# Masking attention scores in place in PSUM with a bitwise AND, in a linear attention kernel with two feed-forward layers

## What is computed

```python
for t in range(S):                       # attention, per batch and head
    kt, vt, rt, wt = (k[:, :, t], v[:, :, t], r[:, :, t], w[:, :, t])
    cur = np.einsum('bhd,bhe->bhde', u[None] * kt, vt)
    y[:, :, t] = np.einsum('bhd,bhde->bhe', rt, state + cur)
    state = wt[:, :, :, None] * state + np.einsum('bhd,bhe->bhde', kt, vt)
...
h = x @ w_in
g = np.maximum(h, 0.0) + alpha * np.minimum(h, 0.0)
x = g @ w_out
...
logits = x @ w_gate                      # then for each expert e, for its tokens:
h = np.maximum(xe @ w1[e], 0.0)
ye = h @ w2[e]
out[mask] = gate_w[mask, None] * ye
```

## Time and profile before

| | us |
|---|---|
| median of 3 runs | 925.89 (922.28 to 926.36) |
| profiled execution, its time | 920.69 |
| its span on the core | 919.0 |
| TensorE busy (matmuls) | 784.9 (85%) |
| VectorE busy | 559.2 (61%) |
| ScalarE busy | 440.3 (48%) |
| POOL busy | 410.0 (45%) |

### The profile page before, as it was taken

The page is one execution under the profiler, slowest core; times in us unless marked ns, Lnnn a source line. Parts: engine busy times, 40 slices in busy tenths (PEclk is TensorE's granted clock), DMA queues, the critical chain, the costliest instruction groups (busy, mean ns, idle before and its releaser), DMA issues.

```text
span 919.0 us, 19098 instructions
## 1 busy us (share of the span) xinstructions
PE 784.9 (85%) x6487; PEld 498.6 (54%) x6488; DVE 559.2 (61%) x1077; ACT 440.3 (48%) x826; POOL 410.0 (45%) x384
## 2 busy tenths in 40 slices
PE   3568979979988988997997997993999999999992
PEld 0364556557556556556556556551555565555551
DVE  8788787787788678868868868213333333333330
ACT  1655756755764763773773773741222222222320
POOL 5305856854963872883973874651001011110100
PEclk9789989999998998998998998996999999999997
DMA  8645552543434335326327324696543415424110
GB/s 256 218 134 133 165 162 75 170 142 96 136 128 144 111 130 168 101 92 213 101 70 229 103 75 148 238 321 230 217 144 95 164 35 183 170 52 166 49 35 14
DMA packets 43372, 128.96 MB, mean 140 GB/s; under 512 B 5632, under 2 KB 26784, under 8 KB 41504
## 3 DMA queue, kind: packets, MB, share of 16 engines
q1 hardware_dynamic: 30656, 105.03, 34.7%
q10 hardware_dynamic: 9120, 12.74, 5.2%
q0 software_dynamic: 3520, 10.17, 2.9%
HBM read 84.92 MB, written 43.78 MB: 140 GB/s over the span
## 4 chain that ended last, share of the span: by engine, by line
PE 40%; POOL 17%; DVE 15%; issue 15%; DMA 7%; ACT 4%; SPq 1%; DVEq 0%; POOLq 0%; ACTq 0%
POOL gl L550 5%; POOL arena L524 5%; PE bank L1511 4%; PE bank L1544 4%; PE bank L1546 4%; PE bank L1513 4%; PE bank L1512 4%; PE bank L1545 4%; DMA arena<-expert_split 4%; DVE att_l L959 3%; POOL shared L493 2%; POOL rk L498 2%; PE bank L1528 2%; DMA rkw_sb<-rkw_dram 2%; PE bank L1433 2%
## 5 line engine op out<-in xcount | busy, mean ns | idle before, releaser
L550 POOL TENSOR_TENSOR gl<-gf,gh 128x384 f16<-128x384 f32 x128 | 121.6, 950 | 119.8 <-ACT gh L680 119.8
L1419 PE MATMUL bank<-xh,arena 128*128 128x384 f16 (+1 forms) x528 | 140.0, 294 | 17.7 <-DVE gf L1133 12.7
L572 POOL DMA_INDIRECT out_dram<-shared,dest x28 | 27.6, 985 | 256.7 <-DVE shared L1237 256.7
L1420 PE MATMUL bank<-xl,arena 128*128 128x384 f16 (+1 forms) x528 | 139.9, 294 | 0.0
L1433 PE MATMUL bank<-arena,gh 128*128 128x392 f16 x384 | 126.8, 330 | 5.0 <-POOL gl L550 5.0
L1434 PE MATMUL bank<-arena,gh 128*128 128x392 f16 x384 | 126.3, 329 | 0.0
L1435 PE MATMUL bank<-arena,gl 128*128 128x392 f16 x384 | 126.3, 329 | 0.0
L524 POOL TENSOR_TENSOR arena<-arena 128x768 f16<-128x768 f32 x64 | 107.8, 1693 | 0.7 <-ACT arena L698 0.7
L1133 DVE SCALAR_TENSOR_TENSOR gf<-neg,slope,bank 128x384 f32<-128x384 f32 x128 | 72.7, 572 | 54.2 <-ACT neg L674 54.1
L680 ACT ACTIVATE gh<-gf 128x384 f16<-128x384 f32 x128 | 66.2, 517 | 63.2 <-DVE gf L1133 63.2
L1422 PE MATMUL bank<-xh,arena 128*128 128x384 f16 (+1 forms) x528 | 95.3, 292 | 0.0
(11 more groups left out here) (180 smaller groups left out, 1854.0 us busy)
## 6 DMA issues: line engine op xcount, KB each, us to landing
arena<-w_exp_dram SPq DMA_DIRECT2D x32, 768.0 KB, 5.9
expert_split<-arena SPq DMA_DIRECT2D x32, 768.0 KB, 4.2
arena<-expert_split SPq DMA_DIRECT2D x8, 3072.0 KB, 10.5
rkw_sb<-rkw_dram SPq DMA_DIRECT2D x64, 144.0 KB, 4.8
route_rows<-pad_rows ACTq DMA_DIRECT2D x8, 788.0 KB, 10.2
shared<-route_rows ACTq DMA_DIRECT2D x31, 197.0 KB, 2.8
rkw_sb<-rkw_dram SPq DMA_DIRECT2D x64, 72.0 KB, 5.1
v_sb<-v_dram SPq DMA_DIRECT2D x8, 576.0 KB, 6.6
```

The costliest lines, as they stand in the source:

```text
L550: pool.tensor_tensor(gl[:, f % 4, :], gf[:, f % 4, :], gh[:, f % 4, :], ALU.subtract).then_inc(gl_done, 1)
L1419: pe.matmul(at, wih[:, k, fs], xh[:, k, lo:hi], start=(k == 0), stop=False)
L1420: pe.matmul(at, wih[:, k, fs], xl[:, k, lo:hi], start=False, stop=False)
```

## The change

`causal`, `att` and their set-up go. In their place a mask `earlier` of 128 x 128 int32 holds -1 (all bits set) where the query is later than the key and 0 elsewhere. VectorE makes a bitwise AND of a score tile with it, broadcast over the four heads, from the PSUM bank into the same bank. ScalarE's high part and VectorE's low part then read the bank. VectorE no longer waits for `att_l_done` ahead of the evacuation, and TensorE's two waits ask for `att_l_done` with the same numbers as for `sc_evac` before. The order of the instructions on every engine is as before; only the memset L891 is gone.

```diff
@@ -84,7 +84,7 @@
-        causal = sb("causal", [128, 4, C], F32)
+        earlier = sb("earlier", [128, C], I32)
@@ -114,7 +114,6 @@
-        att = sb("att", [128, H, C], F32)
@@ -309,6 +308,7 @@
+        heads = lambda tile: tile[:, :].rearrange("p (h t) -> p h t", h=4)
@@ -465,14 +465,14 @@
-            pool.memset(causal[:, :, :], 1.0)
+            pool.memset(earlier[:, :], -1)
...
-            pool.affine_select(out=causal[:, :, :], in_=causal[:, :, :], compare_op=ALU.is_gt, fill=0.0,
-                               base=0, pattern=[[0, 4], [1, C]], channel_multiplier=-1)
+            pool.affine_select(out=earlier[:, :], in_=earlier[:, :], compare_op=ALU.is_gt, fill=0.0,
+                               base=0, pattern=[[1, C]], channel_multiplier=-1)
@@ -614,9 +614,8 @@
-                act.activation(att_h[:, c % 2, 4 * a:4 * a + 4, :], att[:, 4 * a:4 * a + 4, :], ACT.Copy,
-                               scale=QS
-                               ).then_inc(att_h_done, 1)
+                act.activation(att_h[:, c % 2, 4 * a:4 * a + 4, :], heads(b_sc[(2 * c + a) % 3]), ACT.Copy,
+                               scale=QS).then_inc(att_h_done, 1)
@@ -888,7 +887,6 @@
-            dve.memset(att[:, :, :], 0.0)
@@ -945,18 +943,16 @@
-                if not (isinstance(n, int) and n == 0):
-                    dve.wait_ge(att_l_done, 2 * n + a - 1)
                 dve.wait_ge(sc_ready, 2 * n + a + 1)
-                dve.sem_inc(dve_went, 1)
-                dve.copy_predicated(att[:, 4 * a:4 * a + 4, :], causal[:, :, :].bitcast(U32),
-                                    b_sc[q % 3][:, :].rearrange("p (h t) -> p h t", h=4)).then_inc(sc_evac, 1)
+                tile = heads(b_sc[q % 3]).bitcast(I32)
+                dve.tensor_tensor(tile, tile, earlier[:, :].unsqueeze(1).to_broadcast([128, 4, C]), ALU.bitwise_and
+                                  ).then_inc(sc_evac, 1)
 
             def att_low(g, c, a):
...
-                dve.scalar_tensor_tensor(out=att_l[:, c % 2, hd, :], in0=att[:, hd, :], scalar=QS,
+                dve.scalar_tensor_tensor(out=att_l[:, c % 2, hd, :], in0=heads(b_sc[(2 * c + a) % 3]), scalar=QS,
                                          in1=att_h[:, c % 2, hd, :], op0=ALU.mult, op1=ALU.subtract
@@ -1336,7 +1332,7 @@
                 if c >= 1:
-                    pe.wait_ge(sc_evac, 2 * (NC * g + c) - 1)
+                    pe.wait_ge(att_l_done, 2 * (NC * g + c) - 1)
@@ -1402,7 +1398,7 @@
                 pe.wait_ge(xt_evac, UP + NC * g + 1)
-                pe.wait_ge(sc_evac, 2 * NC * (g + 1))
+                pe.wait_ge(att_l_done, 2 * NC * (g + 1))
                 for f in range(3):
                     hidden(g, f, 0, C)
```

## The result

The changed kernel takes 950.2 us (median of 6 runs) against 925.5 us: a ratio of 1.027, 95% interval 1.0248 to 1.0292, so **24.7 us slower**. The profiled execution has a span of 946.3 us against 919.0. The forecast was 945 us, in a range of 934 to 957.

The account below looks back on a forecast made before the run. VectorE was taken to set the pace in attention, TensorE to fill the MLP stage. Eight halves at 2.4 us, the 0.85 us gain included, add 19.2 us to the median 925.9: 945 us, range 934 to 957.

Parts of the forecast that it names:

- The evacuation and the high part: VectorE's 48 ANDs at 0.70 us for copies of 720 ns, ScalarE's high parts 0.03 us shorter each: no effect on time.
- The low part: VectorE's low parts reading PSUM, no longer blocked beside POOL: 2.7 us freed in each of seven halves, 0.85 us arriving.
- scores(g, 2): TensorE's matmuls for these scores wait for a low part until 273.0 us in half 3, fitting before 276.5: no loss.
- hidden: TensorE's three hidden groups in attention wait for the half's last low part and start 2.35 us later.
- 2.4 us per half: Delay up to the third attend, gain already included, given to all eight halves: +19.2 us.
- (c): TensorE's lower clock lasts past the filler through transposes, attend and next hidden: 3.7 us per half, 956 us; chance 0.20.
- (d): The lower clock falls where TensorE waits, the filler runs at the upper: 1.1 us per half, 935 us; chance 0.15.
- (a): TensorE has slack after attend for the filler, only 0.85 us per half arrives: 7 us less, 919 us; chance 0.04.
- (b): VectorE's gain and MLP-stage waits absorb most: 0.8 us per half or less, 926 to 932 us; chance 0.08 within 0.5%.

Follow-up runs that it names:

- and_to_sbuf: Kernel before with only the predicated copy exchanged for a bitwise AND into att in SBUF, waits unchanged: 926.95 us against 927.5, ratio 0.9995.
- wait_hidden: Kernel before with only TensorE's wait ahead of the three hidden calls asking for att_l_done instead of sc_evac: 949.7 us against 919.5, ratio 1.033.
- wait_scores: Kernel before with only TensorE's wait inside scores(g, c), c >= 1, asking for att_l_done instead of sc_evac: 920.5 us, ratio 1.000.
- fill_hidden: Changed kernel plus 24 unread matmuls of 128 columns ahead of TensorE's wait at hidden: 929.3 us against 919.5 for the kernel before, ratio 1.012.
- split_waits: Changed kernel, each of the three hidden calls waiting only for the low part that reads its bank: 927.4 us against 919.5 before, ratio 1.008.
- fill_half: Changed kernel plus 12 unread matmuls ahead of TensorE's wait at hidden: 942.2 us against 925.0 for the kernel before, ratio 1.018.

## Why the prediction was right, and what was mis-sized

**The evacuation and the high part** were costed at nothing: 0.70 us assumed, 686 ns measured; and_to_sbuf shows no effect of the operation. The high part fell by 0.03 us as assumed. Right.

**The low part**: 2.7 us freed, 0.85 to arrive; 0.81 arrive, held back at the instruction named (1.89 us of waiting for the row copies), and POOL's pair of L524 came sooner as said. Right in six of the seven halves. In half 4, where the sum had the same gain, VectorE waits 2.45 us for the row copies, and the last low part ends 0.23 us later than before:

```profile
352.20 0.31 DVE L1007 MAX8 top<-xrow 128x8 f32<-128x8 f32 x3 [2.45 <-ACT xrow L642]
```

wait_hidden minus the change agrees with the gain in time. One reading of the prediction is thin: the earlier trace rows starts only at 269.91 us, so it doesn't show POOL busy beside the L965 at 269.22. What ran there was POOL's L507:

```profile
267.89 2.07 POOL L507 TENSOR_TENSOR cv<-v_sb,c_sb 128x384 f32<-128x384 f32 x2
```

The 48 low parts of 0.67 to 0.69 us, with POOL's L524 beside the first pair in half 3 (274.32 and 274.26 us), settle it.

**`scores(g, 2)`**: start forecast at 273.0 us, measured 283.11 - 272.88 + 262.97 = 273.2 in the scale of before; nothing lost, as forecast. The prediction allowed 2.3 us at half the clock for its 16 matmuls; they took 2.08. wait_scores has 1.000. Right.

**`hidden`**: 2.35 us later forecast, 2.39 measured in half 3 and 2.36 to 2.52 in six halves. In halves 0 and 4, which the sum gave the same, it is 2.89 and 3.43. Right in half 3, 0.3 us per half too small in the mean.

**The step that was mis-sized** is "So I take **2.4 us per half**", with which every half was to lose what half 3 loses up to the third `attend`. The times lost 24.7 us, 3.1 per half. For half 3 the forecast start of the third `attend`, 2.1 to 2.4 us later, holds: 2.26. Three things were put at nothing or taken as equal. The delay of `hidden` is larger in halves 0 and 4. In the even halves the filler can last longer than before: in half 2 the third `attend` follows the first `hidden` after 4.35 us instead of 3.51. And the third `attend` itself takes 1.49 us instead of 1.12 in half 3, because it begins at the lower clock; the sum ended at its start.

Both clock levels stood in the prediction as rivals (c) and (d). The mechanism of (c), that the lower level outlasts the filler, is what half 3 shows, but only in part: it lasts through the transposes and half of `attend`, and the next `hidden` runs at the upper level. In size (c), 3.7 us per half, is about as far from 3.1 as the forecast's 2.4. What (d) describes was not there by itself; fill_hidden makes it. With no lower clock behind the wait the change costs 1.2%, 1.3 to 1.4 us per half, and the lower clock makes up the other 1.5%. That does not mean that the change brought 1.5% of lower clock: most of the filler ran at the lower level in the kernel before too, where it was hidden behind VectorE's low parts, and the late wait put it on the path.

The Trainium skill, "TensorE: Matmul & The Clock Gate", section on oscillation, has it that a wait between bursts makes the next burst start at the lower rate. Here the burst behind the new wait ran mostly at the lower level, but it began at the upper one: its first matmuls take 0.22 us each, and from 293.19 us on they take 0.31.

The traces differ by more than the times, 27.3 us of span against 24.7, and a part of it is not the change's: see the chips in the last section. It doesn't touch the ratios.

**Rival (a)**, slack behind the filler, and **(b)**, absorption in the MLP stage, fell: wait_hidden has +30 us from the wait alone. And the MLP stage absorbs nothing: in the changed kernel half 3 lasts 44.3 us from its first `hidden` of full width (128x384) to the next half's first evacuation, against 44.5 before.

That the measured time lies 5 us above the forecast and inside the range is not luck in the main: the wait, its place and its size in half 3 were forecast, and wait_hidden and split_waits show that it carries the loss. That the range was wide enough for halves 0 and 4 owes something to luck, since it was made for (c) and (d).

## What to carry to other kernels

When an operand moves from a copy into the PSUM bank it came from, the bank is held until its last reader. Look up what TensorE does next with that bank, and who stands ahead of the last reader in its queue; that can cost more than every instruction that became faster. Here a wait per bank and two instructions moved up turned 2.7% slower into 1% faster. And a wait of TensorE has two prices: what it delays, and the clock at which the work behind it then runs. Work that ran at the lower clock for nothing behind another engine pays for it once the wait puts it on the path: here keeping the clock up gave back more than half of the loss.

## What had not been expected of the hardware

- Unread matmuls in front of a wait that is on the path gave back 14 us of 25 (fill_hidden), and half as many gave back somewhat more than half of that (fill_half).
- An instruction of 128x3 elements can be held by POOL. In the changed kernel VectorE's L1021 takes 0.15 us twice, where no L524 of POOL runs beside it. The six other times it takes 1.68 us and ends with POOL's pair of L524, as here in half 3:

```profile
280.62 1.68 DVE L1021 COPY xrow<-token_no 128x3 f32<-128x3 f32 x1
```

```profile
279.03 3.24 POOL L524 TENSOR_TENSOR arena<-arena 128x768 f16<-128x768 f32 x2
```

- The same kernel took 919.5, 925.0 and 927.5 us on three chips. In all four traces from the fastest of them, split_waits and fill_hidden with the in-place form among them, ScalarE starts the first L674 of the MLP stage (L673 in the changed kernel) 1.95 us after its last high part of x in the odd halves, and so it does in the trace of the kernel before. In all traces from the two slower chips, and in that of the changed kernel, it is 2.25 to 3.3 us. So 0.5 to 1.2 us per odd half between the two main traces comes from this and not from the change. What ScalarE waits for there the records do not say, and it was not tried.
